# Three moves in the first MLP run: one operand cast, the order of scratch stores, and the place of three sums

## The reference

```python
for t in range(S):
    state = gamma * state + outer(k[:, :, t], v[:, :, t])
    y[:, :, t] = scale * q[:, :, t] @ state
x = y.transpose(0, 2, 1, 3).reshape(B * S, H * D)
h = np.maximum(x @ w_in, 0.0)            # 512 -> 2048
x = h * h @ w_out                        # 2048 -> 512
xn = x / sqrt(mean(x * x) + 1e-6) * rms_g
g = xn @ w_gate                          # 512 -> 1536
out = (g * sigmoid(g) * (xn @ w_val)) @ w_out2
```

## Time and profile before

| | |
|---|---|
| Time, median of 3 runs | 1065.71 us (1065.6 to 1065.71) |
| Profiled execution, its own time | 1065.43 us |
| Its span, first to last instruction | 1063.7 us |
| TensorE busy | 1053.2 us (99%) |
| VectorE / ScalarE / GpSimd busy | 884.7 / 609.6 / 333.2 us |
| Mean granted TensorE clock | 0.998 |
| TensorE's share of the chain that ended last | 94% |

### The profile page before, as it was taken

One profiled execution on the slowest core, in us unless ns is written; L12 is line 12 of the kernel. 1 busy time (PEld: TensorE's weight loads), 2 busy tenths in 40 slices (PEclk: granted clock), 3 DMA queues, 4 the chain that ended last, 5 costly groups with the idle time before them and its releaser, 6 DMA issues.

```text
span 1063.7 us, 15146 instructions
## 1 busy us (share of the span) xinstructions
PE 1053.2 (99%) x5742; PEld 870.8 (82%) x5742; DVE 884.7 (83%) x935; ACT 609.6 (57%) x879; POOL 333.2 (31%) x244
## 2 busy tenths in 40 slices
PE   8999999999999999999999999999999999999999
PEld 6886888888888888888888888888888888888887
DVE  5888889878879878789799998977886986978696
ACT  4865675557664667664674645646454555544453
POOL 1827551004540005430035554005544102544000
PEclk9999999999999999999999999999999999999999
DMA  9999568763438644365642335632225751140456
GB/s 366 413 415 397 195 230 271 220 209 126 183 127 264 212 144 173 139 238 198 217 160 100 119 119 217 206 132 74 66 61 145 269 198 60 43 119 21 136 193 186
DMA packets 82759, 195.74 MB, mean 184 GB/s; under 512 B 30584, under 2 KB 39416, under 8 KB 75648
## 3 DMA queue, kind: packets, MB, share of 16 engines
q1 hardware_dynamic: 76960, 189.74, 51.4%
q10 hardware_dynamic: 5728, 5.04, 1.4%
HBM read 152.17 MB, written 42.48 MB: 183 GB/s over the span
## 4 chain that ended last, share of the span: by engine, by line
PE 94%; DMA 3%; DVE 1%; POOL 1%; SPq 0%; issue 0%; ACTq 0%; ACT 0%; POOLq 0%
PE Y L897 13%; PE Y L898 13%; PE Y L899 13%; PE Z L897 9%; PE Z L899 9%; PE Z L898 9%; PE X L897 9%; PE X L898 9%; PE X L899 9%; DMA qkv_sb<-qkv 2%; DMA raw_w<-w_b 1%; PE Z L848 1%; PE X L819 1%; DVE ops L1402 1%; PE Y L819 1%; PE R L872 1%
## 5 line engine op out<-in xcount | busy, mean ns | idle before, releaser
L742 POOL TENSOR_TENSOR w_ops<-raw_w,w_ops 128x512 fp32r<-128x512 f32 x90 | 128.7, 1430 | 487.7 <-ACT w_ops L1026 487.5
L1090 ACT CAST ops<-hid 128x1024 fp32r<-128x1024 f32 x147 | 154.6, 1054 | 155.4 <-PE Y L899 53.3
L1490 DVE TENSOR_TENSOR ops<-hid,ops 128x1024 fp32r<-128x1024 f32 x147 | 179.7, 1225 | 37.7 <-ACT ops L1090 37.3
L742 POOL TENSOR_TENSOR w_ops<-sums_w,w_ops 128x512 fp32r<-128x512 f32 x120 | 167.4, 1398 | 122.8 <-ACT w_ops L1026 122.3
L897 PE MATMUL Y<-ops,w_ops 128*128 128x512 f32 x360 | 140.4, 390 | 0.4 <-DVE ops L1402 0.4
L899 PE MATMUL Y<-ops,w_ops 128*128 128x512 f32 x360 | 140.1, 389 | 0.0
L898 PE MATMUL Y<-ops,w_ops 128*128 128x512 f32 x360 | 140.1, 389 | 0.0
L1115 ACT ACTIVATE gt<-gt 128x512 f32<-128x512 f32 x72 | 45.1, 632 | 111.7 <-DVE gt L1710 38.9
L897 PE MATMUL Y<-ops 128*128 128x512 f32 (+1 forms) x264 | 100.3, 380 | 0.0
L898 PE MATMUL Y<-ops 128*128 128x512 f32 (+1 forms) x264 | 100.1, 379 | 0.0
L899 PE MATMUL Y<-ops 128*128 128x512 f32 (+1 forms) x264 | 100.1, 379 | 0.0
(11 more groups left out here) (182 smaller groups left out, 2251.2 us busy)
## 6 DMA issues: line engine op xcount, KB each, us to landing
ops<-item_scratch SPq DMA_DIRECT2D x147, 512.0 KB, 3.7
raw_w<-w_f SPq DMA_DIRECT2D x30, 1024.0 KB, 5.0
qkv_sb<-qkv SPq DMA_DIRECT2D x17, 1024.0 KB, 8.6
item_scratch<-hid SPq DMA_DIRECT2D x30, 512.0 KB, 3.1
y_scratch<-hid SPq DMA_DIRECT2D x12, 512.0 KB, 6.0
raw<-y_scratch SPq DMA_DIRECT2D x3, 2048.0 KB, 9.2
raw<-w_b SPq DMA_DIRECT2D x5, 1024.0 KB, 5.1
out<-hid SPq DMA_DIRECT2D x36, 128.0 KB, 5.3
```

The source lines that it names most:

```text
L742: nc.gpsimd.tensor_tensor(w_ops[:, k, 1], front_w_source(m, k), f32(w_ops[:, k, 0]), ALU.subtract).then_inc(w_lo, 1)
L1090: nc.scalar.copy(hop_at(bk, n)[:, 0], hid[:, 2 * g:2 * g + 2, OPERAND[k], :])\
L1490: nc.vector.tensor_tensor(hop[:, 1], hid[:, 2 * g:2 * g + 2, OPERAND[k], :], f32(hop[:, 0]), ALU.subtract).then_inc(own_lo if bk.own_place ...
```

## The change

1. `high_front(0, 3)` moves from run 0 into attention, behind ScalarE's casts for chunk 21. A wait is added ahead of `combine(0, 3)` on VectorE (`front_lo` 3).
2. The six stores of held chunks move from ScalarE's queue to SyncE's. There they stand behind the stores of the items 6 to 11, and the store of item 0 moves from ahead of item 7 to between the second and third of them. ScalarE waits for `y_copied` 24 ahead of `seed(0)`.
3. In `first_run` the order becomes seed, high 4, save_p5, item cast, high 5, save_u2, high 6, `high_w(1, 0)`. `high_w(1, 0)` now follows high 6.
4. The three `sum_w` of run 1 move on VectorE from slot 1 to slot 2, behind `low_front(0, 5)`.

```diff
--- before.py
+++ after.py
@@ -495,6 +495,11 @@
                 dst = item_dram[7 * quad + i].rearrange("p (l d) -> p l d", l=2)
                 sp.dma_start(dst, f32(item_at(quad, i))).then_inc(kept_by(quad, i), 16)
 
+            def store_held(n):
+
+                i = stored_chunks().index(divmod(n, CH))
+                sp.dma_start(x_dram[i].rearrange("p h k t -> p (h k t)"), stored_y(n)).then_inc(x_stored[i % 3], 16)
+
             load_first_qk(0)
             load_first_qk(1)
             load_first_kv(0)
@@ -522,7 +527,15 @@
                 store_item(0, i)
             sp.wait_ge(quad_lo, 7)
             load_raw_w(1)
-            for i in (6, 0, 7, 8, 9, 10, 11, 1, 2, 3, 12, 13):
+            for i in range(6, 12):
+                store_item(*divmod(i, 7))
+            sp.wait_ge(y_copied, NCH)
+            for n in (NCH - 3, NCH - 2):
+                store_held(n)
+            store_item(0, 0)
+            for n in (HELD, HELD + 1, HELD + 2, NCH - 1):
+                store_held(n)
+            for i in (1, 2, 3, 12, 13):
                 store_item(*divmod(i, 7))
 
             def load_items(bk, lo, hi):
@@ -1166,15 +1179,15 @@
 
             def first_run():
 
+                act.wait_ge(y_copied, NCH)
                 seed(0)
-                high_front(0, 3)
+                high_front(0, 4)
+                save_p5(0)
                 high_quad(1, 6)
-                save_p5(0)
-                high_front(0, 4)
+                high_front(0, 5)
                 save_u2(0)
-                high_front(0, 5)
+                high_front(0, 6)
                 high_w(1, 0)
-                high_front(0, 6)
                 act.wait_ge(*done(0, 3))
                 nc.scalar.activation(hid[:, 0:2, A, :], X[:], ACT.Relu).then_inc(relu_x, 1)
                 for k in range(1, 5):
@@ -1337,13 +1350,10 @@
                     high_w(0, 2 * n - 9)
                 for quad, i in early_casts(n):
                     high_quad(quad, i)
-                if n in (4, 13, 19):
-                    high_front(0, (4, 13, 19).index(n))
+                if n in (4, 13, 19, 21):
+                    high_front(0, (4, 13, 19, 21).index(n))
                 if n < HELD:
                     store_x(n)
-                elif n == NCH - 1:
-                    for held in range(HELD, NCH):
-                        store_x(held)
             for t in range(TILES):
                 bk = BackRun(t, False)
                 for p in range(R1):
@@ -1441,6 +1451,8 @@
                     op = nc.vector.tensor_tensor(raw_slot(Bb), raw_slot(Dd), raw_slot(Bb), ALU.subtract)
                 else:
                     dve.wait_ge(front_t, 4 * front + 2)
+                    if front == 0:
+                        dve.wait_ge(front_lo, 3)
                     op = nc.vector.tensor_tensor(raw_slot(A), raw_slot(C), raw_slot(A), ALU.subtract)
                 op.then_inc(front_t, 1)
 
@@ -1583,7 +1595,7 @@
                     low_front(front, 3 + slot)
                     if slot == 0 and front == 0:
                         combine(front, 3)
-                if m == 0 and slot == 1:
+                if m == 0 and slot == 2:
                     sum_w(1, 0)
                     sum_w(1, 2)
                     sum_w(1, 1)
```

## The result

The changed kernel takes 1067.17 us (median of 21 runs, 1065.87 to 1068.53), the kernel before 1065.29 beside it (21 runs, 1064.21 to 1066.05). The ratio is 1.0019, 95% interval 1.0012 to 1.0026: slower by 1.9 us. I had forecast 1065.5 and no change. The interval leaves no change out, and the sign is the other one than in my sum of -0.1 us. The profiled execution took 1066.89, its span is 1065.1 us (before 1063.7).

The account below looks back on a forecast made before the run. It took VectorE's chain ahead of product 6 in run 0, sharing turns with GpSimd, as the bound. Turns -0.8 and clock +0.7 gave -0.1 us, 1065.6 against median 1065.71, rounded to 1065.5; 8-in-10 range 1062.2 to 1067.4.

Parts of the forecast that it names:

- my sum of -0.1 us: Whole change: -0.8 us for the turns ahead of product 6 plus +0.7 us for TensorE's clock.
- The sum on the port: Run 0: VectorE and GpSimd take turns on SBUF inputs, filling 17.0 of 17.1 us; product 6 at 103.9 or 102.7.
- the case with 55 in 100: GpSimd's first low weight gets its turn before VectorE's second sum: product 6 at 103.9, -0.3 us.
- the clock term of the sum: Low clock after TensorE's idle ahead of product 6: bounds 0 and 1.7 us, taken 1.0 less 0.3: +0.7 us.
- I take -0.8: Turn order ahead of product 6 in run 0: -0.3 or -1.5 us, weighted 55 to 45.
- The 0.3 taken off for before: Part of the kernel before's low clock not hidden under the wait for `c22_done`, subtracted from the 1.0 us.
- rival C: Whole low-clock stretch falls behind product 6's start at 103.9 or later: +1.1 us, 1066.8; 2 in 100 beyond 0.2%.
- A: Sums, even low 6, pass ahead of GpSimd; product 6 at 101.6 or 100.4: 1062.8 to 1061.6 us; 22 in 100.
- B: SyncE's full queue delays the load of run 2's weights to 114.6; run 1's product 6 waits 4.6 us: 1070; 8 in 100.

Follow-up runs that it names:

- e2: The changed kernel with the six held stores back on ScalarE's queue and item 0's store in its old place; ratio 0.9974, 1062.69 us.
- e6: The changed kernel with one added wait: GpSimd begins run 1's low weights only after VectorE's low 6; ratio 0.9971, 1062.65 us.
- e5: The changed kernel with ScalarE's cast of the last weight item behind high 5 instead of ahead of it; ratio 0.9997, 1065.78 us.
- e1_fill: The changed kernel with 15 extra matmuls, results unused, between products 5 and 6 of run 0; ratio 1.0006, 1065.8 us.
- e7_before_pool_waits: The kernel before with only one wait added: GpSimd begins run 1's low weights after VectorE's low 6; ratio 0.9976, 1063.09 us.
- e3: The kernel before with only the three sums of run 1 moved behind low 5; ratio 1.0003, 1065.95 us.
- e8: The kernel before with only high 3 moved into attention and the added wait ahead of the combine; ratio 0.9989, 1064.65 us.
- e9: The kernel before with 8 extra matmuls, results unused, between products 4 and 5 of run 0; ratio 0.9999, 1065.83 us.
- e4: The changed kernel with the three sums of run 1 moved further, behind the line of `c22_done`; ratio 0.9990, 1063.98 us.

## Why the prediction was wrong

**The sum on the port: right.** GpSimd's sum ended at 91.54 (91.6 in the prediction), high 5 at 93.21 (93.25), low 5 at 95.12 (95.15), low 6 at 101.43 (101.5), product 6 began at 103.74 (103.9). GpSimd got the first turn, the case with 55 in 100. Experiments e2 and e6 take its turns out of the chain and win 3.3 and 3.2 us at product 6; e5 makes an operand 2 us earlier and wins 0.8 there.

**The step that failed is the clock term of the sum.** "I take 1.0", less 0.3, gave +0.7; product 6 became 1.5 us longer, twice that. The other open term, "I take -0.8" for the turns, came out at -0.4, half of it. So instead of cancelling to -0.1 they left run 1 1.0 us later. How the clock term was mis-sized: a low stretch costs 1.7 us where all of it lies on matmuls, and of that 1.7, 1.7 and 1.4 us came in the three profiles (4.44, 4.44 and 4.19 us for product 6, against 2.75). In two of them the clock fell 0.5 to 0.7 us after TensorE had resumed, in the third about 0.5 us before, so that a small part was spent in the idle. The row I had pointed there: resumed at 99.78, low from 101 on the earlier trace rows. I averaged in two cases, no fall at all and a stretch wholly inside the idle. No profile of this kernel shows either, and by the mean clock one of its 33 executions had no fall. The 0.3 taken off for before was too much as well: product 6 took 2.96 there, 0.2 over 2.75, and in 51 of 83 executions there was no low stretch to take off. Averaging was the second fault: the likelier turn order with the whole stretch exposed gives -0.3 - 0.3 + 1.7 = +1.1, 1066.8, the number of rival C, to which I gave 2 in 100 only because I asked for more than 0.2% from it.

**What is left of the 1.9 us.** Run 1 starts 1.0 us later, and the lag is still 1.07 at 151 us (the same product starts at 150.66 before and at 151.73). The profiled executions differ by 1.46 (1066.89 against 1065.43); the 0.3 to 0.4 that come after 151 us have no cause that I can name. The remaining 0.42 is between profile and median: the profiled execution of before lies 0.14 over its median, that of the changed kernel 0.28 under its own. Part of this is the clock: seven of 21 executions had more of the low clock than the profiled one, and theirs are the seven longest times. Where those stretches lie is not known, since none was profiled. Nor is the clock all of the scatter: e1_fill has 1.000 in every execution and still 2.4 us between lowest and highest, e2 and e6 1.1 and 0.6.

**Rivals.** A happened, in e2_act_stores, by the very mechanism (the store of item 11 landing after 94.5), with product 6 at 100.45 where I had worked out 100.4 for no turn at all; in the changed kernel the store landed in 2.6 us and shut it out. B did not: the load of run 2's weights was issued at 100.22 and landed at 108.4, 2.4 us after the later end of my 104.6 to 106, but was needed at 110.66. Each issue ahead of it took 0.6 to 1.2 us; whether that is the whole reason is not shown. C is what came: +1.1 worked out, +1.0 at run 1, +1.9 in the median.

## What to carry to other kernels

When two engines take turns on one resource and its turns fill the time, starting one of them earlier moves little (4.7 us here moved product 6 by 0.4); count the turns that lie ahead of the wait that ends last, and take those out that are not needed there. Look also at what delays the other engine's request by chance: here a slow store did the ordering, and removing it cost more than the rest of the change won, while one explicit wait brought 0.24% to the kernel before (0.9976, e7_before_pool_waits) and took the changed kernel from 1.0019 to 0.9971 (e6_pool_waits). Gather idle of TensorE only where the work behind it is hidden: two pieces of 0.4 and 2.2 us, with the low clock behind them under the wait for `c22_done`, were cheaper than one of 3.8 with the low clock behind it on exposed work. And take a profile as one execution: where the clock falls in some executions only, the mean clock of each says which kind was profiled.

## What the runs showed of the hardware

An idle of TensorE did not always bring the clock down: 2.87 us (e3), 2.88 (e5) and 1.40 (e8, e9) did not in the profiled execution, 2.23 (before), 1.97 (e4) and 3.8 (three times) did. By the mean clock the changed kernel, with 3.8 us, had no fall in 1 of 33 executions, e5 in 2 of 11, e3 in 3 of 11, e4 in 7 of 11 and the kernel before in 51 of 83.

VectorE and GpSimd took turns on inputs in SBUF: a sum of VectorE took 0.68 us with no turn of GpSimd ahead (e2) and 1.75 to 1.77 with one (changed kernel), low 6 1.22 and 2.30.

A DMA of 512 KB issued at the same moment, 89.3 us, landed after 2.6 us in the changed kernel, where from 89.0 to 89.64 only SyncE's queue moved data, and after 6.1 us in e2_act_stores, where in the same stretch ScalarE's queue moved 0.14 MB beside 0.11 of SyncE's.
